# Block sums of a head pair computed beside its own first scores and copied out by ScalarE, in a windowed-attention and mixture-of-experts kernel

## The reference, cut to what matters

```python
block, window = (32, 16)
nb = S // block                                   # 24
k_sum = k.reshape(B, H, nb, block, D).max(axis=3)
v_sum = v.reshape(B, H, nb, block, D).mean(axis=3)
scores_l = scale * q @ k^T, masked to |i - j| < window
scores_s = scale * q @ k_sum^T + log(block)
a = softmax over the concatenation [scores_l, scores_s]
v_all = np.concatenate([v, v_sum], axis=2)
return np.matmul(a, v_all)
```

## Time and profile before

| what | us |
|---|---|
| median of 3 runs | 379.94 |
| the profiled execution, its own time | 379.92 |
| its span in the profile | 378.2 |
| TensorE matmul busy | 326.6 (86%) |
| VectorE busy | 175.9 (47%) |
| ScalarE busy | 143.6 (38%) |
| GpSimd busy | 101.1 (27%) |
| last weighted values of attention start | 121.84 |

### The profile page before, as it was taken

How to read it: one execution, slowest core, us unless ns; L and a number is a source line. 1 busy time by engine, 2 the same in 40 slices (tenths; PEclk the granted TensorE clock), 3 DMA queues, 4 the chain that set the end, 5 groups by cost and what they waited for, 6 DMA issues and landing times.

```text
span 378.2 us, 9016 instructions
## 1 busy us (share of the span) xinstructions
PE 326.6 (86%) x3272; PEld 233.9 (62%) x3273; DVE 175.9 (47%) x406; ACT 143.6 (38%) x329; POOL 101.1 (27%) x181
## 2 busy tenths in 40 slices
PE   0879879889898999969877795999999999999991
PEld 0556656667677754232325264788888888888880
DVE  2577867877885553360116596132331323213231
ACT  1476666666876422310110262123232322313221
POOL 5665675676764000000000000121211212112121
PEclk9999999999999999987998999699999999999996
DMA  7999999999999716999942900110101111010110
GB/s 306 362 425 408 414 423 415 419 419 420 410 385 406 297 50 227 383 390 405 393 156 83 364 2 0 57 47 36 55 28 55 41 42 55 28 55 34 49 56 32
DMA packets 23851, 81.64 MB, mean 216 GB/s; under 512 B 2312, under 2 KB 2312, under 8 KB 21776
## 3 DMA queue, kind: packets, MB, share of 16 engines
q1 hardware_dynamic: 20640, 73.08, 49.1%
q0 software_dynamic: 1920, 6.29, 4.4%
q10 hardware_dynamic: 1264, 1.92, 1.5%
HBM read 74.99 MB, written 6.29 MB: 215 GB/s over the span
## 4 chain that ended last, share of the span: by engine, by line
PE 57%; DMA 16%; DVE 11%; ACT 4%; POOL 4%; issue 4%; SPq 2%; ACTq 0%; DVEq 0%; POOLq 0%
PE ps L904 33%; DMA ring<-in_vt 11%; DMA ring<-in_moe_w 5%; PE ps L630 3%; POOL ring L503 3%; PE ps L643 3%; PE ps L890 3%; PE ps L600 3%; ACT work L962 2%; PE ps L787 2%; SPq L285 2%; PE ps L746 2%; DVE ps L1128 2%; PE ps L651 1%; PE ps L709 1%
## 5 line engine op out<-in xcount | busy, mean ns | idle before, releaser
L904 PE MATMUL ps<-high_w2b,hid_high 128*128 (+1 forms) x184 | 73.1, 397 | 4.1 <-DVE hid_low L1372 4.1
L904 PE MATMUL ps<-low_w2b,hid_high 128*128 (+1 forms) x184 | 72.8, 396 | 0.0
L904 PE MATMUL ps<-high_w2b,hid_low 128*128 (+1 forms) x184 | 72.5, 394 | 0.0
L962 ACT ACTIVATE work<-ps,small 128x120 f32<-128x120 f32 x192 | 53.9, 368 | 39.3 <-DVE small L1132 39.1
L556 POOL DMA_INDIRECT out_x<-work,small x24 | 23.6, 982 | 150.2 <-DVE small L1365 61.5
L1372 DVE SCALAR_TENSOR_TENSOR hid_low<-ps,hid_high 128x1024 fp32r<-128x1024 f32 x26 | 31.8, 1225 | 57.3 <-ACT hid_high L1062 57.3
L1044 ACT ACTIVATE work<-ps,small 128x512 f32<-128x512 f32 x24 | 16.5, 689 | 99.0 <-PE ps L904 99.0
L904 PEld LDWEIGHTS ps<-high_w2b,hid_high 128*128 128x128 f32 x184 | 35.3, 192 | 11.6 <-issue 4.5
L600 PE MATMUL ps<-ident,work 128*120 128x128 f32 x192 | 31.8, 289 | 10.8 <-ACT work L962 10.6
L904 PEld LDWEIGHTS ps<-high_w2b,hid_low 128*128 128x128 f32 x184 | 35.2, 191 | 7.5
L904 PEld LDWEIGHTS ps<-low_w2b,hid_high 128*128 128x128 f32 x184 | 35.3, 192 | 7.0
(11 more groups left out here) (230 smaller groups left out, 368.7 us busy)
## 6 DMA issues: line engine op xcount, KB each, us to landing
ring<-in_moe_w SPq DMA_DIRECT2D x13, 2048.0 KB, 13.4
ring<-in_qk SPq DMA_DIRECT2D x16, 1104.0 KB, 14.5
ring<-in_v SPq DMA_DIRECT2D x16, 780.0 KB, 10.1
ring<-in_moe_w SPq DMA_DIRECT2D x10, 512.0 KB, 11.3
ring<-in_vt SPq DMA_DIRECT2D x7, 384.0 KB, 8.8
comb<-in_vt SPq DMA_DIRECT2D x7, 384.0 KB, 8.2
x_or_g<-in_moe_w SPq DMA_DIRECT2D x1, 2048.0 KB, 9.0
whole_w2b<-in_moe_w SPq DMA_DIRECT2D x4, 512.0 KB, 9.0
```

The lines of the kernel that those rows point to most:

```text
L904: last = pe.matmul(ps[:, 4 + u, :], hidden_part[:, u, m * P:(m + 1) * P], matrix[:, bass.ds(e * UNIT + m * DM, DM)], start=m == 0 and i == ...
L962: last = act.activation(probs[u][:, j, :], sc[u][:, j // 2, (j % 2) * KC:(j % 2 + 1) * KC], ACT.Exp, bias=negmax[u][:, j:j + 1], scale=flo ...
```

## The change

The matmul that makes the block sums of pair n (n > 0) moves on TensorE: out of the first step of pair n - 1, to stand directly ahead of pair n's own first scores, behind the wait for `gaps_filled`. Its output goes to an unused corner of the bank that these scores use. The copy to `vsum` moves from VectorE to ScalarE, behind the four exponentials of that first step of pair n. Pair 0 stays on VectorE with a semaphore of its own (`first_vsum`). On GpSimd `fill_sums(0)` now stands ahead of `halve(1)`; for the later pairs its order stays.

```diff
-        block_sums = [av[u][3 * SLAB:4 * SLAB, BANK - P:BANK] for u in range(2)]
+        first_sums = av[0][3 * SLAB:4 * SLAB, BANK - P:BANK]
+        block_sums = [flat[3 * SLAB:4 * SLAB, 2 * u * BANK + BANK // 2:2 * u * BANK + BANK // 2 + P] for u in range(2)]
...
             def fill_sums(n):
                 b, pair = n // NPAIR, n % NPAIR
-                pool.wait_ge(vsum_ready, n + 1)
+                if n:
+                    pool.wait_ge(vsum_ready, n)
+                else:
+                    pool.wait_ge(first_vsum, 1)
...
             fill_gaps(0)
+            fill_sums(0)
             halve(1)
-            fill_sums(0)
             for n in range(1, B * NPAIR):
...
+            def sums_by_block(to, pair):
+                pe.matmul(to, vb[pair % 2], ident[:, :], start=True, stop=True, tile_position=(0, 3 * SLAB),
+                          skip_group_check=True).then_inc(vsum_done, 1)
             def scores(b, s):
                 if g == 0:
                     pe.wait_ge(gaps_filled, b * NPAIR + pair + 1)
                     pe.sem_inc(pair_started, 1)
+                    if not (isinstance(b, int) and b * NPAIR + pair == 0):
+                        pe.wait_ge(vb_ready, b * NPAIR + pair)
+                        sums_by_block(block_sums[u], pair)
...
             def weighted_values(b, s):
...
-                if g == 0:
-                    ahead_pair(sums_by_block, b, pair + 1, u)
...
             scores(0, 0)
-            sums_by_block(0, 0, 0)
+            pe.wait_ge(first_vb, 1)
+            sums_by_block(first_sums, 0)
...
             def exps(b, s):
                 last.then_inc(exp_done, 1)
+                if s % NG == 0 and not (isinstance(b, int) and b * NSTEP + s == 0):
+                    n = b * NPAIR + s // NG
+                    act.wait_ge(vsum_done, n + 1)
+                    act.wait_ge(sums_filled, n)
+                    act.activation(vsum[3 * SLAB:4 * SLAB, 1:1 + P], block_sums[u], ACT.Copy).then_inc(vsum_ready, 1)
...
-            def copy_block_sums(b, pair, u):
-                dve.wait_ge(vsum_done, b * NPAIR + pair + 1)
-                dve.tensor_copy(vsum[3 * SLAB:4 * SLAB, 1:1 + P], block_sums[u]).then_inc(vsum_ready, 1)
...
             def attended(b, s):
-                if g == 0:
-                    ahead_pair(copy_block_sums, b, pair + 1, u)
...
-            copy_block_sums(0, 0, 0)
+            dve.wait_ge(vsum_done, 1)
+            dve.tensor_copy(vsum[3 * SLAB:4 * SLAB, 1:1 + P], first_sums).then_inc(first_vsum, 1)
```

More of the change, by code:

```diff
@@ L222, in attention_soft_moe_switch_moe @@
         vT_loaded = [sem(f"vT_loaded{u}") for u in range(2)]; vb_ready = sem("vb_ready"); first_vb = sem("first_vb")
-        vsum_done = sem("vsum_done"); vsum_ready = sem("vsum_ready"); sums_filled = sem("sums_filled")
+        vsum_done = sem("vsum_done"); vsum_ready = sem("vsum_ready"); first_vsum = sem("first_vsum"); sums_filled = sem("sums_filled")
         kmax_ready = sem("kmax_ready"); gaps_filled = sem("gaps_filled"); pair_started = sem("pair_started"); top_seq = sem("top_seq")
@@ L601, in probs_T @@
                 last.then_inc(pT_done, 1)
[L603 to L615, removed]
             def weighted_values(b, s):
```

## The result

The changed kernel takes 404.62 us, the median of 4 runs (403.8 to 405.66); the kernel before 379.88 over its 4. The ratio is 1.065, with a 95% interval from 1.061 to 1.068: slower by 24.7 us. The forecast was 402.9 with a range from 399 to 408.

What follows compares the result with a forecast made beforehand. A ring of TensorE, VectorE and ScalarE was taken to set 6.63 us a pair, with GpSimd 1.77 to spare. Fourteen turns of 8.47 from 16.05 put attention's end 23.0 later: 379.92 becomes 402.9, range 399 to 408.

Steps and rivals of the forecast that it cites:

- The ring: From one fill_gaps end to the next, through sums, scores, exponentials, ScalarE's copy, fill_sums and halving: a new closed path.
- Its size: One pair's turn in attention: 8.47 us instead of 6.63, with GpSimd idling 3.61 instead of 1.77.
- the row that I took: ScalarE's copy of the sums: 0.37 us, taken from its 128x120 copy as the nearest in length.
- The assumed overlap: ScalarE behind the exponentials: the copy can start 0.13 us before the last one ends, so at 3.12.
- The sum: Pair 1's gaps end at 16.05, 14 turns of 8.47 follow; exponentials 22.8 us later, plus 0.24 in the tail: 23.0.
- The clock: Rival: TensorE's clock falls while it idles, 1.04 us more a turn, 14.6 in all, so 417.5; chance 0.03.
- the 1.04 of the rival: Extra time of sums and scores in a turn if TensorE ran at 1.2 instead of 2.4 GHz.
- Loads: Transfers of transposed values have 14.1 us against 12.4 for the slowest; the 5.0 of waits disappear into longer turns.
- The start's swap: At the start, fill_sums(0) begins at 11.19 and pair 1's gaps end at 16.05; earlier weighted values gain nothing.
- The faster rival: GpSimd's spare time swallows the detour, each turn is 0.33 us shorter, 5.0 in all: 374.9; chance 0.03.
- The rule that was cited with it: Where VectorE is saturated, handing work to ScalarE may make sense; by it the change gains.
- The signs: In the new profile: fill_sums waits some 3.6 us 15 times, TensorE idles 1.5 or more a pair, later work shifts 23.

Runs made afterwards that it cites:

- e1: Changed kernel with GpSimd doing halve(n + 1) ahead of fill_sums(n) for pairs 1 to 15; 381.31 us, ratio 1.0032 against the kernel before.
- e3: Changed kernel with ScalarE's copy ahead of the pair's first exponentials and the matmul writing to the weighted values' bank; 379.96 us, ratio 1.001 against the kernel before.
- e8: Changed kernel with the copy back on VectorE, ahead of the row maxima, and the matmul writing to the weighted values' bank; 380.36 us, ratio 1.000.
- e2: Changed kernel with ScalarE's copy of the sums one instruction later, behind the copy of the turned probabilities; 414.88 us, ratio 1.092 against the kernel before.
- e9: Changed kernel with the matmul back in its old place, ahead of the weighted values of the pair before; 410.58 us, ratio 1.080 against the kernel before.
- e10: Changed kernel with eight dummy matmuls on TensorE ahead of its wait for the gaps; 405.18 us, ratio 1.066 against the kernel before.
- e5: Changed kernel with halve(1) ahead of fill_sums(0) again, the start's reordering undone; 404.7 us, ratio 1.067 against the kernel before.
- e4: Kernel before with only fill_sums(0) put ahead of halve(1); 380.09 us, ratio 1.0007.
- e7: Changed kernel with halve(n + 1) ahead of fill_sums(n) and ScalarE's copy behind the copy of the turned probabilities; 380.11 us, ratio 1.0014 against the kernel before.

## Why the prediction was right, point by point

**The ring.** The step that decided was that the copy now hangs on exponentials that hang on `fill_gaps(n)`, with the next halving queued behind it. It is shown from four sides: another order on GpSimd removes the loss (e1), so does an earlier copy (e3, e8), a later copy adds to it one for one where the clock is up (e2), and neither the matmul's place (e9) nor the clock (e10) makes it.

**Its size.** 8.47 was forecast and 8.52 measured. Two errors cancelled in part: the copy took 0.27 and not 0.37 (0.10 less), and it started 0.03 behind the last exponential and not 0.13 ahead of it (0.16 more). The estimate by the Trainium skill's price (ScalarE: Activation LUTs, What ACT_TABLE_LOAD costs) was 293 ns; the trace has 272 on the mean, so the page came nearer than the row that I took. The assumed overlap was taken from a copy of 120 partitions; why this one of 32 partitions does not overlap was not tried.

**The sum.** The span grew by 24.8 and not 23.0. By its steps:

- Step 45's exponentials start at 138.51, 24.55 later than before, with 22.8 forecast. 0.14 is the first load's landing, 0.77 is 13 turns of 0.06 more, and 0.84 is the first turn, 25.08 - 15.77 = 9.31.
- That first turn was not walked through on its own. TensorE was still at its lower clock there: the scores' 16 matmuls took 1.01 and the sums 0.64 (0.58 and 0.38 later), both on the ring. The scores ended 1.95 after the gaps and not 1.16, which is nearly all of the 0.84. In the kernel before the sums of that turn, at 15.49, took 0.38; why the higher clock came later here was not looked into.
- From step 45's exponentials to the last weighted values it is 9.00 (147.51 - 138.51) against 7.88, with 0.24 of difference forecast. In the window from 138 to 142 the granted clock is 0.62:

```profile
138.00:142.00 4.00, 4.00 (x60) 3.00 (x58) 1.88 (x6) 2.33 (x8) 1.80 (x3) 0.62 0.52 207
```

TensorE had sat idle for 2.00 just before the sums at 136.53. In e10, with the clock at 1.00, the same stretch takes 8.21 (147.44 - 139.23), so 0.8 of the 0.88 too much is the clock's.

- What follows attention took 0.9 less, and what lies around the span 0.4 more. Neither was looked into. The 0.9 is luck: it hid a part of the miss in attention.

**The clock.** I held that it would not fall, and it did (0.90 to 0.91 on the mean from 24 to 134). I had excluded it by one stretch of before with 1.44 of idle time in it. From pair 3 on it falls in every second turn, after 1.92 to 2.00 of idle time in one piece; in the turns between, the idle time is 0.8 to 0.9 and it stays up. In pair 2 it stayed up after 1.92 too. One such turn:

```profile
102.36 0.38 PE L579 MATMUL ps<-ident,small 128*32 128x128 f32 x2 [1.92 <-POOL ring L496]
...
102.79 0.58 PE L602 MATMUL ps<-ring 64*64 64x120 f32 x16
...
103.31 0.96 PE L611 MATMUL ps<-ident,work 128*120 128x128 f32 x4
```

The sums and scores, which are on the ring, are still at the higher clock; the transposes behind them are the first at the lower one. So the clock cost some 0.8 in the first turn and 0.8 at the end, and not 14.6. That it falls just behind the scores and not on them is luck. The traces of e5, e2 and e9 have it on the scores in 3, 5 and 7 turns behind the first, and there it makes a turn up to 0.9 longer, near the 1.04 of the rival. Where in a turn it falls was not forecast and is not explained here.

**Loads.** Right: no wait for transfers in the longer turns.

**The start's swap.** Right: nothing (e4, e5).

**The faster rival.** Its condition, `fill_sums` within 1.44 of the gaps, was not met even in e3, with 1.80. What it promised, 5.0, was wrong as well: with GpSimd out of the way the move to ScalarE gives 0.08 a turn (e1), or 0.22 with the copy one place later (e7), and not 0.33. The rule that was cited with it (the Trainium skill, Perfetto Trace Analysis, Optimizing Scalar/DVE Operations) speaks of a saturated VectorE, and at 10.61 of 13.60 busy it is open whether this one was. By itself it did not tell where the time would go: ScalarE's queue was on the same chain as VectorE's.

**The signs.** `fill_sums` waited some 3.66 for 14 of the 15 pairs, as said there. Wrong was that TensorE idles 1.5 or more in each (0.8 to 0.9 in every second), and that all behind attention shifts by 23 (25.7, less the 0.9).

## What to carry to other kernels

Before an instruction is moved to another engine, walk the ring that it closes: what it waits for there, what that waits for, and what is queued behind whoever waits for its result. An engine with 27% in the page can be the one that decides, if an in-order queue puts a long step of the next round behind a short one of this round; changing that order took back 23 of 25 us. And a shorter turn is worth its time only down to the next floor, here in part the transfers, so look for loads that can go later.

## What the runs showed of the hardware that was not expected

- ScalarE's copy of 32x128 from PSUM took 272 ns on the mean, less than VectorE's 299 for the same shape. It started 0.02 to 0.03 after the instruction ahead of it had ended, in the changed kernel (behind exponentials) and in e2 and e3 (behind a 120x512 copy), while the 120x512 copy behind the exponentials starts 0.13 before their end.
- TensorE's granted clock dropped to a mean of 0.62 from 138 to 142 (its two levels are 1.2 and 2.4 GHz) after an idle time of 2.00, and in every second turn after 1.92. With dummy matmuls in that gap (e10) it stayed at 1.00 from 24 to 147. In kernels that differ little, the fall came behind the scores (the changed kernel) or on them (e5, three turns).
